# Pooled-query attention with a feed-forward stage on one core: VectorE inverts the softmax sums behind the step's row maximum

## What is computed

```
q_pool = q.reshape(B, H, S // 2, 2, D).mean(axis=3)
scores = scale * q_pool @ k.T
attn = exp(scores - max(scores)); attn = attn / (sum(attn) + 1e-09)
x = (attn @ v), heads side by side: 2304 tokens x 512
h = x @ w_in;  g = max(h, 0) + alpha * min(h, 0);  out = g @ w_out
```

## Time and profile before

| what | value |
|---|---|
| median of three runs | 896.88 us |
| the profiled execution | 897.15 us |
| its span in the trace | 895.4 us |
| PE busy | 856.4 us, 96% |
| PE weight loads busy | 611.2 us, 68% |
| VectorE busy | 511.9 us, 57% |
| ACT busy | 421.7 us, 47% |
| GpSimd busy | 204.9 us, 23% |
| granted TensorE clock, mean | 0.998 |
| row maxima (L489) | 144 of 1353 ns |
| slot copies on VectorE (L523) | 144 of 685 ns |
| inverts | 32 of each of three instructions, 0.15 to 0.21 us |

### The profile page before, as it was taken

One profiled execution on the slowest core, in us unless ns is written; L12 is line 12 of the kernel. 1 busy time (PEld: TensorE's weight loads), 2 busy tenths in 40 slices (PEclk: granted clock), 3 DMA queues, 4 the chain that ended last, 5 costly groups with the idle time before them and its releaser, 6 DMA issues. The chain is left out here.

```text
span 895.4 us, 19923 instructions
## 1 busy us (share of the span) xinstructions
PE 856.4 (96%) x6577; PEld 611.2 (68%) x6577; DVE 511.9 (57%) x786; ACT 421.7 (47%) x935; POOL 204.9 (23%) x170
## 2 busy tenths in 40 slices
PE   3899999999999999999999999999999999999996
PEld 1455555555555555555557998998899998999985
DVE  1777777777776767777774434435443445344442
ACT  1666666666666666666663222224222224222222
POOL 2111111101011010111312232233223223322320
PEclk9999999999999999999999999999999999999999
DMA  7436443554346453563222222213221222222211
GB/s 190 121 93 153 94 122 92 147 130 114 99 111 151 108 128 84 134 151 92 67 81 62 71 59 59 69 59 115 75 70 59 61 68 99 91 59 70 59 35 71
DMA packets 42638, 84.37 MB, mean 94 GB/s; under 512 B 7536, under 2 KB 15728, under 8 KB 42608
## 3 DMA queue, kind: packets, MB, share of 16 engines
q1 hardware_dynamic: 40208, 79.28, 33.9%
q10 hardware_dynamic: 2400, 4.72, 1.6%
HBM read 79.18 MB, written 4.79 MB: 94 GB/s over the span
## 5 line engine op out<-in xcount | busy, mean ns | idle before, releaser
L683 PE MATMUL slot_ps<-ff 128*128 128x384 f32 x1152 | 218.0, 337 | 1.4 <-PEq L680 1.4
L489 DVE TENSOR_REDUCE neg_max<-s_ps 128x1 f32<-128x1152 f32 x144 | 194.8, 1353 | 30.5 <-DVEq L488 29.7
L683 PEld LDWEIGHTS slot_ps<-ff 128*128 128x128 f32 x1152 | 204.3, 188 | 11.2 <-issue 3.2
L699 PE MATMUL s_ps<-ff 128*128 128x512 f32 x720 | 182.4, 394 | 2.2 <-PEq L696 2.2
L604 PE MATMUL s_ps<-k_f,q_f 64*128 64x512 f32 (+1 forms) x640 | 161.1, 632 | 6.3 <-PEq L615 5.2
L399 ACT ACTIVATE e_sb<-s_ps,neg_max 128x1024 f32<-128x1024 f32 x144 | 159.7, 1109 | 0.0
L631 PE MATMUL pv_ps<-pt,v_f 128*64 128x256 f32 (+1 forms) x1152 | 155.1, 412 | 0.2 <-PEq L650 0.2
L699 PEld LDWEIGHTS s_ps<-ff 128*128 128x128 f32 x720 | 133.4, 188 | 26.6 <-issue 3.7
L631 PEld LDWEIGHTS pv_ps<-pt,v_f 128*64 128x64 f32 x1152 | 76.7, 136 | 95.8 <-issue 52.6
L330 POOL TENSOR_TENSOR q_raw<-q_raw 128x576 f32<-128x576 f32 x32 | 44.9, 1402 | 358.2 <-POOLq L329 358.2
L541 DVE TENSOR_SCALAR e_sb<-slot_ps,alpha_sb 128x384 f32<-128x384 f32 x96 | 59.3, 618 | 114.6 <-DVEq L539 114.6
(11 more groups left out here) (32 smaller groups left out, 504.6 us busy)
## 6 DMA issues: line engine op xcount, KB each, us to landing
q_raw<-in_q SPq DMA_DIRECT2D x64, 288.0 KB, 4.0
k_f<-in_k SPq DMA_DIRECT2D x64, 288.0 KB, 4.2
wi_raw<-in_w_in SPq DMA_DIRECT2D x48, 256.0 KB, 2.6
wo_raw<-in_w_out SPq DMA_DIRECT2D x48, 256.0 KB, 2.6
v_f<-in_v SPq DMA_DIRECT2D x32, 288.0 KB, 3.7
out<-pt ACTq DMA_DIRECT2D x6, 768.0 KB, 3.9
inv_bc<-sums SPq DMA_DIRECT2D x32, 80.0 KB, 3.6
k_end<-in_k SPq DMA_DIRECT2D x64, 32.0 KB, 3.9
```

Of the source, the lines that this page charges most:

```text
L489: nc.vector.tensor_reduce(out=neg_max[:, b:b + 1], in_=s_ps[:, S_AT[b]:S_AT[b] + NKEY], op=ALU.max, axis=AX_X, negate=True).then_inc(max_r ...
L683: ins = nc.tensor.matmul(slot_ps[h][:, 0:TOK], w[i][:, d * P:(d + 1) * P], x[h][:, d * TOK:(d + 1) * TOK], start=(d == 0 and w is wi_hi an ...
L699: ins = nc.tensor.matmul(y_ps[h][t], g[h][:, t * P:(t + 1) * P], w[i], start=(first == 0 and j == 0), stop=(last == 1 and j == 2))
```

## The change

The call of `invert` moves from between the copy of slot 1 and the copy of ninth blocks to behind the row maximum, the last thing of a step. `INVERT` becomes a table for each g: group 0 stays at t = 5 for both, group 1 stays at t = 0 for g = 1 (s = 9) and moves from t = 0 to t = 1 for g = 0 (s = 18 to s = 19). In the very last step, which has no row maximum, group 1 is inverted behind the copy of ninth blocks. No instruction is added or removed.

```diff
-    INVERT = {5: 0, 0: 1}
+    INVERT = [{5: 0, 1: 1}, {5: 0, 0: 1}]
...
@@ step on VectorE @@
                     nc.vector.tensor_copy(pt_half((s - 1) % TILES, 1),
                                           half_columns(slot_ps[1][:, :])).then_inc(slot_free[1], 1)
-                if t in INVERT and (INVERT[t] == 0 or pair is not None):
-                    invert(INVERT[t])
                 if s % 2 == 0:
...
                     row_max(s + 2)
+                if t in INVERT[g] and (INVERT[g][t] == 0 or pair is not None):
+                    invert(INVERT[g][t])
+                elif left < 0:
+                    invert(1)
```

## The result

| | before | changed |
|---|---|---|
| median of 11 runs | 897.01 us (896.19 to 897.83) | 899.01 us (898.32 to 899.67) |
| ratio of changed to before | | 1.0022, 95% interval 1.0013 to 1.0031 |
| span of the profiled execution | 895.4 us | 897.2 us |

The change makes the kernel 2.0 us slower, against a forecast of +1.4 and a range of 895.0 to 900.2. The loss is small, 0.2%, but the interval of the ratio leaves out 1. First the waits of PE after the change; columns as in the earlier trace rows.

What follows compares the result with a forecast made beforehand. The attention stage was taken as bound by PE, except where PE waits for what VectorE releases. Terms -0.58 + 0.45 + 1.5 = +1.4 us on the 896.88 median gave 898.3 us, range 895.0 to 900.2.

Steps and rivals of the forecast that it cites:

- The loop's end: Step 23, seven times: 0.70 us won at PE's ninth transposes becomes a wait for the slot copy; together +0.45 us.
- the 3.91 of the first body: Time between PE's half-transpose starts of steps 24 and 25, first loop pass; usually 3.52, the excess blamed on PE's loop branch.
- The first pair: Step 5, ahead of the loop: no scale follows the invert, so the earlier row maximum gains; -0.58 us.
- s = 9: Eight times, the moved invert delays scale and slot copy, so PE starts step 11 later by 0.19; +1.5 us.
- s = 14 and 18 to 19: Invert moves costed at 0: PE's own work covers the first with 0.3 us to spare, the second has 0.5.
- the rule that a delay of T stays to the end: T(s), PE's weight-load start for step s's half transposes: delays or gains persist unless a later stall is fixed to something else.
- The gap ahead of the scale: On VectorE, from the invert's turn to the next scale's start: taken as 0.36 us, lower end 0.15.
- Rival 1: The moved invert costs VectorE only its own durations and PE keeps the gain: -3.0 us, 893.9; chance 0.14.
- Rival 2: The invert's turn stays late, delaying scale and slot copy at s = 23 and 9: up to 1.7 more, 900.0; chance 0.22.
- The upper bound: The turn held at 0.76 behind the first invert instruction instead of 0.64, in fourteen places: +1.7 us, 900.0.
- Rival 3: Step 14's spread transfer lands late and holds step 18's scale; one such us more gives 906; chance 0.03.

Runs made afterwards that it cites:

- the two spare inverts: The changed kernel plus an extra invert, its results unread, behind the real one: in step 14, 903.53 us; in step 19, 900.42 us.

## Why the prediction was right

- *The loop's end.* Forecast: the 0.70 at the ninth transposes won, then a wait for the slot, +0.10 a time and +0.45 in all. Measured 0.70 won, +0.12 a time in most and +0.7 in all. The first body gave -0.27 (forecast -0.29), the last +0.26 (+0.24). The rest of the difference is two of the middle bodies with +0.16 and +0.17, and 0.02 a time that the scale was later. One reading was wrong, though no term of the sum hangs on it: the 3.91 of the first body was put down to PE's branch. Of the 0.39 over the usual 3.52, 0.25 lie ahead of the ninth transposes, where VectorE's turn came 0.70 behind the reciprocal instead of 0.46; only 0.14 lie between them and T(25), where the branch is.
- *The first pair.* Forecast -0.58, measured -0.57.
- *s = 9.* Forecast 8 x 0.19 = +1.5, measured +1.5. The sum is met partly by luck: +0.18 or +0.19 came in step 10 six times but only 0.10 and 0.09 the first and last time, and 0.2 in step 11, for which nothing was forecast, made up for it. For the last time the forecast took the scale's gap at 0.36 with its register operation, which is not there behind the loop (0.26).
- *s = 14 and 18 to 19.* Forecast 0, measured 0; the two spare inverts show covers of about 0.5 in both places. My working of the first was too small by 0.2, and the rule that a delay of T stays to the end was too general: behind T(21) most of it is given back.
- *The gap ahead of the scale.* Forecast 0.36 between bounds of 0.15 and 0.36 and more, measured 0.36. Rival 1 (the invert costs its own durations) is out: by its price T(25) would have come 0.2 earlier. Between two instructions of the invert it is 0.30 and 0.34 from start to start for 0.15 and 0.19 of work, while the spare sum of step 14, which waits for nothing, starts 0.14 behind a turn of 0.21. The Trainium skill (VectorE: DVE Perf Modes, The DRAIN you can't avoid) found that the semaphore between VectorE copies in a chain costs nothing extra; for instructions this short, each dependent on the last, the trace does not agree. How much of the gap is the semaphore and how much the dependence no run here separates.
- *Rival 2* (the turn stays late) is out: it came 0.34 behind the reciprocal at the loop's end, not 0.46, so the old delay belonged to the place in the program; the runs that leave this invert in its old place have it again (0.46 in six bodies). The upper bound counts fourteen places for this delay; there are fifteen, seven loop ends and eight steps 9, which moves it by 0.1. *Rival 3* is out: every scale of step 18 starts 1.48 behind the row maximum, before and after, although the turn in step 14 comes 2.1 us later.
- The sum came out at 2.0 for 1.4. Of the 0.6, about 0.25 is the loop ends'. The two profiles differ by 1.8, of which the places named make 1.6, so the other 0.35 is single steps, the start, and the distance of the profiled executions from the medians, at the size of the runs' spread; no cause is shown for it. The forecast had the result just below 1.8 us, the line between no change and slower by 0.2%, and it came just above.

## What to carry to other kernels

When an instruction is moved out of one wait's way, follow the same engine's queue to the next thing that someone waits for: here, counted from the slot copy of the step, the row maximum came 0.6 to 0.7 us earlier and the next slot copy, behind invert and scale, 0.3 to 0.4 later, and PE waited for whichever was last. Two moves that are each worth less than nothing (a late invert +2.0; a late scale +4.7, of which 1.7 is two held instructions) were worth -6 together, so a change that only relocates a stall is a reason to look for its partner, not to drop it. Where a schedule is tight to 0.1 us, a small VectorE instruction with two SBUF inputs can fall onto a GpSimd operation as soon as the rhythm shifts; give it one operand from SBUF if that is possible.

## What the runs showed of the hardware

- A VectorE instruction with two SBUF inputs of 4 or 5 elements a row took 1.41 us instead of 0.15 when a GpSimd addition of two SBUF inputs had begun 0.04 us before it, and 2.27 when a GpSimd subtraction of 3.44 us was in progress. When it had begun first it took 0.15, and with one input it took 0.15 beside the same operation.
- The start-to-start distance of VectorE instructions of 0.15 to 0.19 us, each waiting for the last, was 0.30 to 0.34. Behind a turn of 0.21 us that nobody on the engine waits for, the next instruction started after 0.15 with one wait ahead of it, 0.26 or 0.27 with two, and 0.36 with two and a register operation.
- Between the ninth transposes and T(25), where PE's loop branch lies, it was 1.16 us in the first body, 1.02 in a middle one and 0.89 at the exit, for the same work.
